# Attention, gated FFN and mixer in one Trainium2 program: one way of normalising for every head pair, 65-column V weights, and a re-timed order of late copies

## The reference

```python
def _attn_ref(q, k, v, s):                       # B, H, S, D = 4, 8, 576, 64
    scores = scale * np.matmul(q, k.transpose(0, 1, 3, 2))
    cum = np.cumsum(np.maximum(s, 0.0), axis=-1)
    bias = -(cum[:, :, :, None] - cum[:, :, None, :])
    scores = np.where(causal, -1e9, scores + np.minimum(bias, 0.0))
    attn = np.exp(scores - scores.max(-1, keepdims=True))
    attn = attn / (attn.sum(-1, keepdims=True) + 1e-09)
    return np.matmul(attn, v)
...
def _moe_ref(x, w_in, conv_w, w_out):            # 512 -> 1024 -> 512
    h = np.maximum(x @ w_in, 0.0)
    conv_out = sum(conv_w[k] * shifted(h, k - 1) for k in range(3))
    return (h / (1 + np.exp(-conv_out))) @ w_out
...
def _moe2_ref(x, U, V, w_ch1, w_ch2):            # rank 32; 512 -> 2048 -> 512
    u = x + (x.transpose(0, 2, 1) @ U @ V).transpose(0, 2, 1)
    return u + np.maximum(u @ w_ch1, 0.0) @ w_ch2
```

## Time and profile before

| | |
|---|---|
| median of 3 runs | 921.22 us (920.56 to 921.58) |
| the profiled execution | 922.75 us, its span 921.0 us |
| PE busy | 873.2 us (95%) |
| DVE, ACT, POOL busy | 483.6, 373.2, 41.6 us |
| mean granted TensorE clock | 0.98 |
| DMA | 149.14 MB, mean 162 GB/s |

### The profile page before, as it was taken

One profiled execution on the slowest core, in us unless ns is written; L12 is line 12 of the kernel. 1 busy time (PEld: TensorE's weight loads), 2 busy tenths in 40 slices (PEclk: granted clock), 3 DMA queues, 4 the chain that ended last, 5 costly groups with the idle time before them and its releaser, 6 DMA issues.

```text
span 921.0 us, 15633 instructions
## 1 busy us (share of the span) xinstructions
PE 873.2 (95%) x6184; PEld 831.9 (90%) x6184; DVE 483.6 (53%) x992; ACT 373.2 (41%) x709; POOL 41.6 (5%) x85
## 2 busy tenths in 40 slices
PE   4888898989999999999999999999999999999998
PEld 3676898879999999898999999988999999999998
DVE  6778794554448843554335871356225670442222
ACT  2667584654425634544233553444121431321110
POOL 3020000000000000000000000000000000000000
PEclk9979899989999999999999999999999999999999
DMA  7679356634764356435544453444243434355441
GB/s 161 167 211 308 111 149 204 217 79 149 239 200 173 131 190 200 153 115 198 174 153 144 144 170 113 166 128 163 92 151 140 181 138 177 144 189 182 145 177 52
DMA packets 63628, 149.14 MB, mean 162 GB/s; under 512 B 29514, under 2 KB 43850, under 8 KB 51012
## 3 DMA queue, kind: packets, MB, share of 16 engines
q1 hardware_dynamic: 61252, 144.50, 47.8%
q0 software_dynamic: 2304, 3.65, 1.7%
HBM read 117.97 MB, written 30.09 MB: 161 GB/s over the span
## 4 chain that ended last, share of the span: by engine, by line
PE 82%; DVE 8%; issue 4%; ACT 4%; DMA 1%; POOL 0%; DVEq 0%; ACTq 0%; POOLq 0%
PE psum L1170 22%; PE psum L1172 21%; PE psum L1171 21%; PE psum L1151 7%; PE psum L1098 3%; PE psum L1130 2%; PE psum L1128 2%; DVE psum L875 1%; PE psum L1135 1%; DVE work L942 1%; DMA spread_out<-few_scratch 1%; PE psum L1111 1%; ACT qc L675 1%; PE psum L1225 1%; DVE sums L895 1%
## 5 line engine op out<-in xcount | busy, mean ns | idle before, releaser
L1170 PE MATMUL psum<-uu_hl,ring 128*128 128x288 f32 x512 | 156.6, 306 | 7.6 <-DVE u_acc L997 2.9
L1170 PE MATMUL psum<-r_hl,ring 128*128 128x288 f32 x512 | 154.5, 302 | 1.9 <-DVE u_acc L997 1.1
L1172 PE MATMUL psum<-uu_hl,ring 128*128 128x288 f32 x512 | 152.8, 298 | 0.0
L1171 PE MATMUL psum<-uu_hl,ring 128*128 128x288 f32 x512 | 152.6, 298 | 0.0
L1172 PE MATMUL psum<-r_hl,ring 128*128 128x288 f32 x512 | 151.1, 295 | 0.0
L1171 PE MATMUL psum<-r_hl,ring 128*128 128x288 f32 x512 | 151.0, 295 | 0.0
L985 DVE SCALAR_TENSOR_TENSOR r_hl<-psum,r_hl 128x288 fp32r<-128x288 f32 x128 | 58.4, 457 | 133.9 <-ACT r_hl L773 133.9
L773 ACT ACTIVATE r_hl<-psum 128x288 fp32r<-128x288 f32 x128 | 52.4, 410 | 183.3 <-PE psum L1172 183.2
L1151 PE MATMUL psum<-probs,va 128*128 128x320 f32 (+4 forms) x448 | 117.4, 383 | 6.2 <-ACT probs L681 6.2
L875 DVE CUSTOM_DVE_ANT_0 psum<-psum,key_late 128x512 f32<-128x512 f32 (+4 forms) x160 | 84.7, 564 | 60.6 <-PE psum L1098 60.1
L1170 PEld LDWEIGHTS psum<-uu_hl,ring 128*128 128x128 f32 x512 | 97.8, 191 | 11.2 <-DVE u_acc L997 4.2
(11 more groups left out here) (104 smaller groups left out, 1654.1 us busy)
## 6 DMA issues: line engine op xcount, KB each, us to landing
ring<-w_scratch SPq DMA_DIRECT2D x74, 1024.0 KB, 4.8
w_scratch<-ring SPq DMA_DIRECT2D x24, 1024.0 KB, 6.1
...
spread_out<-few_scratch POOLq DMA_DIRECT2D x24, 144.0 KB, 4.3
...
```

The source lines that it names most:

```text
L1170: pe.matmul(o, hi, m_hi, start=start, stop=False)
L1171: pe.matmul(o, hi, m_lo, start=False, stop=False)
L1172: return pe.matmul(o, lo, m_hi, start=False, stop=stop)
```

## The change

1. `va` holds 64 columns of V and one of ones; `values` multiplies with 65 columns, outputs are always on partitions 0 to 63 and the sums on partition 64. ACT copies them to the half that the head has in its pair.
2. Pair 3 is normalised like the others (`invert_few`, `normalise_few`; POOL gathers, stores and spreads four pairs instead of three). The direct form is gone. Positions: batch 0's last pair is inverted in step (0, 1) of batch 1, multiplied in (0, 4), split in (1, 0); in batches 2 and 3 inverted in (0, 0), multiplied in (0, 1), split in (0, 2); in `END` at items 2, 5 and 6. In batch 1 the FFN begins 3 attention steps later.
3. `TURN` is [3, 3], and in batches 1 to 3 the transposes stand behind `values` of that step.
4. ACT: `y_high` and `weights_high` of the last item of a step (`follow`) come behind the attention part of the next step.
5. DVE: `x_low` of pairs 0 to 2 moves from ahead of a step's FFN items to behind them.
6. `order`: no pair in the middle of wi; one pair stands behind "split" (the last low part of u), ahead of "up".
7. SP: the third `load_small` two steps sooner; POOL clears two columns of each of the two parts of `hid`, not all 1156.

```diff
+        SMALL_AT = {(0, 4): 0, (1, 4): 1, (2, 2): 2}
...
-        TURN = [3, 4]
+        TURN = [3, 3]
...
             for f in range(FT):
                 seq.extend(pair("wi", b, f))
-                if f == FT // 2:
-                    fill(1)
...
                 fill_between(*([("mix", b, 0, d, half) for d in range(KT)] for half in range(2)))
+                seq.append(("split", b, 0, KT - 1, 0))
+                fill(1)
...
-        PLAN = {a: spread(BESIDE[a], len(ATT_STEPS) - 3 * (a == 1), 3 * (a == 1), a == 1) for a in BESIDE}
+        PLAN = {a: spread(BESIDE[a], len(ATT_STEPS) - 6 * (a == 1), 6 * (a == 1), a == 1) for a in BESIDE}
...
-        END_NORMALISE = (0, 1)
-        END_SPLIT = 2
+        END_INVERT, END_NORMALISE, END_SPLIT = 2, 5, 6
...
-        X_SPLIT_LAST = [{}, {(0, 2): (NPAIR - 2, NPAIR - 1)}, {(0, 2): (NPAIR - 1,)}]
+        X_SPLIT_LAST = [{}, {(0, 2): (NPAIR - 2,), (1, 0): (NPAIR - 1,)}, {(0, 2): (NPAIR - 1,)}]
+
+        NORMALISE = [(4, 6), (3, 5, 7)]
+        INVERT_LAST = [(0, 1), (0, 0)]
+        NORMALISE_LAST = [(0, 4), (0, 1)]
...
-                    for pair in range(NPAIR - 1):
+                    for pair in range(NPAIR):
...
-                            pool.memset(hid[:, :, :], 0.0).then_inc(s_hid, 1)
+                            pool.memset(hid[:, :, 0:S + 2:S + 1], 0.0).then_inc(s_hid, 1)
...
-                    if h // 2 == 1:
-                        norm.wait(act, m - 2)
...
+                    if m >= 2:
+                        few_in.wait(act, m - 2)
+                    act.activation(sums[sm:sm + 1, h // 2 % 2, :], psf[D:D + 1, O0:O0 + S], ACT.Identity, bias=EPS)\
+                       .then_inc(evict.sem, 1)
...
+                def follow(item):
+                    kind, b, unit, i, half = item
+                    if kind == "wi" and half and i:
+                        y_high(b, i - 1)
+                    for of, q in REFILL.get(item, ()):
+                        if made(of, q):
+                            weights_high(q)
+
+                def body_step(a, h, g):
+                    attention_step(a, h, g)
+
+                    if STEP_BEFORE.get((a, h, g)):
+                        follow(STEP_BEFORE[a, h, g][-1])
...
-                    if a and (h, g) in X_SPLIT[1]:
-                        x_low(a, X_SPLIT[1][h, g])
...
+                    if a and (h, g) in X_SPLIT[1]:
+                        x_low(a, X_SPLIT[1][h, g])
...
-                        mm = pe.matmul(psf[:, O0 + i0:O0 + i1], va[i][:, t, :], probs[:, c % 2, at:at + w],
+                        mm = pe.matmul(psf[0:D + 1, O0 + i0:O0 + i1], va[i][:, t, 0:D + 1], probs[:, c % 2, at:at + w],
```

More of the change, by code:

```diff
@@ L788, in ffn_step @@
                         hidden(b, i, half)
-                        if i:
-                            y_high(b, i - 1) if half else gate(b, i - 1)
+                        if i and not half:
+                            gate(b, i - 1)
                     if kind == "gated":
@@ L802, in ffn_step @@
                         hidden2(b, unit, i, half)
[L803 to L805 removed]
+                    if item not in LAST_OF_STEP:
+                        follow(item)
                 for h in range(2):
```

74 lines of the change are left out of this document (32 added, 42 removed).

## The result

The changed kernel takes 911.37 us (median of 6 runs) against 920.89 us (median of 6 runs) for the kernel before in the same job: a ratio of 0.9905, 95% interval 0.9878 to 0.9932. It is faster, by 9.5 us (6.3 to 11.2 by the interval) where 23 were forecast. The profiled execution took 910.87 us, its span 909.1.

What follows compares the result with a forecast made beforehand. PE, busy 873.2 of 921.0 us, was taken as the bound, so only its waits, clock and own instructions count. Terms sum to -23.1 us from 922.75, giving 899.7, stated as 898 for the median; range 888 to 913.

Steps and rivals of the forecast that it cites:

- Small loads and memset: Batch 0, near 51 us: sooner loads and less clearing end 2.5 us of PE waiting and 3.5 of low clock, -6.0 us.
- 65 columns: Values products of all heads: half of the exposed weight load, 4 us in all, goes, -2.0 us.
- Batch 0 to 1: Last pair at that change: waits of 1.6 and 2.0 us and 0.5 for clock against 5.1 before, -1.0 us.
- Exponentials ahead: Batch 1, last wi tile: wait of 2.37 us ends, but DVE still owes its work; -1.0 of a possible -3.1 us.
- Turn sooner, `x_low` later: Batch 1: PE's waits of 1.6 and 1.64 us and a low stretch of 3.5 go, 1.0 may stay, -5.7 us.
- Batches 2 and 3: Mixing there: waits from `x_low` and `uu_hl` go, 6.5 us, with low stretches of 1.3 and 3.1, -10.9 us.
- The last pair there: Batches 2, 3 and `END`: gathered pair's transfers make DVE wait 3.3 us and PE 1.5 at each start; sum +2.2 us.
- DVE becomes the bound in wi: Rival: DVE needs 3.65 us a wi tile against PE's 3.2, all four wi runs lose; +12, 910 us, chance 0.22.
- The clock falls anyway: Rival: new short gaps close together bring low clock; two thirds of the 11.4 us taken back stay, 906 us, chance 0.15.
- The change does not do what it says: Rival: a removed wait was only the last of several; the mixing's gaps stay at half, +8, 906 us, chance 0.06.

Runs made afterwards that it cites:

- e4: Kernel before, with the third `load_small` two steps sooner and only the edges of `hid` cleared: 915.1 us, ratio 0.9944.
- e15: Changed kernel, third convolution tap in batch 0's FFN on an eighth of its columns, late copies ahead of the exponentials again: 911.1 us, ratio 0.9882.
- e7: Kernel before, with sooner small loads, only the edges of `hid` cleared, and `x_low` of pairs 0 to 2 behind the FFN items: 911.5 us.
- e16: e11 with the direct inversion ahead of pair 2's multiplication after batch 0, and the transposes in step 3 behind `values`: 908.1 us, ratio 0.9856.
- e17: Changed kernel with parts 3 and 4 undone (old turn, late copies ahead of the exponentials), gathered last pair kept: 911.6 us, ratio 0.9891.
- e11: Kernel before with parts 5, 6 and 7 and 65 columns for six of eight heads; without parts 2, 3 and 4: 906.3 us, ratio 0.9827.
- e14: Changed kernel with part 2 undone: last pair inverted directly, 128 columns for heads 6 and 7, FFN of batch 1 three steps sooner: 911.8 us.
- the light convolution: Changed kernel with the third convolution tap in batch 0's FFN computed on an eighth of its columns: 912.9 us, ratio 0.9909.
- the square: Four kernels with or without part 2 and parts 3 with 4: e11 906.3 us, e14 911.8, e17 911.6, the changed kernel 911.4.
- e1: Changed kernel with part 3 undone, the transposes in step 4 ahead of `values` again: 913.6 us, ratio 0.9899.
- e2: Changed kernel with part 4 undone, late copies ahead of the next step's attention on ACT again: 912.1 us, ratio 0.9906.

## Why the prediction was right and wrong

The direction was right, the size was not. Profile against profile the sum said -23.1 us and 11.9 came. By batch: batch 0 -6.5 said, -4.4 came; batch 1 -8.2 said, **+0.8** came; batches 2, 3 and `END` -8.4 said, -8.3 came. So the prediction failed in batch 1. Of the 9.0 us there the waits and the low stretches (at 0.34 us per us), an estimate from the rows, place 1.5 in the change of batch, 2.3 at the last wi tile and 3.5 in the mixing; 1.7 are not placed.

- **Small loads and memset: right.** 6.2 us by the median of e4 against 6.0, though its interval (3.0 to 7.4) is too wide to show more than the size. The low clock near 51 us is gone from both profiles, the gap there is 1.03 us in e4 and 0.64 in the changed kernel, and DVE's copy takes 0.45 us where it took 1.40 beside the clearing, the 0.95 that was said.
- **65 columns: right in size**: 1.9 us by the loads and some 2.8 by the stages, against 2.0; the medians put it at 3.4 to 4.2, with an uncertainty as large as the difference.
- **"Batch 0 to 1": wrong, by size.** Waits of 1.6 and 2.0 us and 0.5 for the clock were said; 3.17 and 0.99 us stand there, and a low stretch of 6.8 us behind them (2.3 us at 0.34). The transfers were sized rightly: 6.3 to 11.0 us from the issue of the store to the multiplication, where 2.0 to 6.6 and 4.3 were said. That DVE's wait for pair 2 holds up the maxima was said too; it was priced at half of what it took. An estimate from the Trainium skill ("DMA: Bandwidth & Descriptors", Anatomy of one DMA: 2.0 us and bytes over 436 GB/s for each transfer) gives 4.4 us for the store and a spread of 144 KB behind it. The store alone is near that in the changed kernel (1.7 us); the two together are not, with 6.3 us there and 11.0 us in e15, where other transfers were in flight.
- **"Exponentials ahead": wrong in its price and in most of its mechanism.** It said that DVE owes the work whatever ACT does, and kept 1.0 of 3.1 us. The wait came back whole (3.25 for 2.37), and with it a low stretch of 3.4 us that was not there before. Taking 3.6 us of work from DVE left it at 3.0, putting the copies first again at 2.79, and both together at 1.71: the last tile goes through DVE and ACT in turn, and part 4 put ACT's share of it behind exponentials that wait for PE. The prediction named that second cause, but left it without a price.
- **"Turn sooner, `x_low` later", batch 1: wrong in its mechanism, the largest miss.** "Both causes go" was true, word for word: no wait for `qc`, no `x_low` ahead of the mix. But 0.73 (`row_max`), 1.45 (`ybuf`), 0.83 (mix half) and 1.83 us (exponentials) stand where 1.0 (`ybuf`), 0.5 (mix half), 1.6 and 1.64 stood, so of -5.7 us only the shorter low stretch is left, some 2 us. A cause that ends last was priced as if nothing came just ahead of it. The experiments tell which part did it: part 5 alone took the waits for `ybuf` and the mix half away (e7). Part 3, priced as the end of a 1.6 us wait, brings them back (e16), with a median 2.7 us higher, and so does part 2 without part 3 (e17: 1.27 and 1.00 us for `ybuf`).
- **Batches 2 and 3: right in sum, for a wrong reason, so by luck.** The waits and the moved pair were said to give -6.5 and +1.3, of which -1.2 and +1.3, so nothing, was part 6's; e7 and e11 give -3.7 and -2.6 in those stages, so part 5 was overpriced and part 6 was a gain. The 4.4 us of clock were in the profiled execution, but e4 lost them with no edit there.
- **The last pair there: right.** +2.2 said; part 2 costs 1.4 to 1.9 us in those stages (e11 to e17, e14 to the changed kernel). DVE waited 1.95, 1.85 and 3.94 us for `spread_out`; 3 was said.
- Not in the sum at all: parts 3 and 4 cost 1.5 to 2.0 us in batches 2, 3 and `END`, where the text gave them nothing.

That the medians differ by 9.5 us where the profiles differ by 11.9 goes with the clock: over all executions some 15 us less at 0.50, an estimate from the granted clocks, against 24 us in the two profiles. At 0.34 us each that is 3 us.

Of the rivals, "DVE becomes the bound in wi" gave 910 us and came nearest in time, but its mechanism does not stand: in batches 2, 3 and `END` wi shows waits of 0.6 to 0.7 us, and in batch 1 the light convolution refutes it. "The clock falls anyway" gave 906 us and is in part what happened: three stretches of 13.7 us are left, all in batch 1, behind new waits that add up to what the old ones did. "The change does not do what it says, one of the removed waits was only the last of several" is what happened in batch 1; it had 0.06 and 906 us, and placed the miss in the mixing's gaps.

What stays open: why parts 2 and 3 with 4 cost 5 us each where the other is away and nothing more together. The traces show different waits in batch 1 for each (above), but a single execution's stage moves by up to 4 us with the clock and the transfers, so how batch 1 shares in the square is not shown beyond the estimate there. Parts 3 and 4 were not told apart in it beyond e1, e2 and e16.
